# Second mixture-of-experts stage: one check of the routing search at the end instead of one per phase, and the low parts of w1 and w2 made by other engines and by adding DMAs

## The reference

```python
N, D, E, F = 3072, 512, 8, 1024
cap = N // E                                  # 384
logits = x @ w_gate                           # [N, E]
for idx in argsort(-logits.flatten()):        # all (token, expert) pairs, highest first
    tok, e = idx // E, idx % E
    if assigned[tok] >= 0 or counts[e] >= cap: continue
    assigned[tok] = e; counts[e] += 1
for e in range(E):
    mask = assigned == e                      # exactly 384 tokens
    out[mask] = np.maximum(x[mask] @ w1[e], 0) @ w2[e]
```

## Time and profile before

| | |
|---|---|
| time, median of 3 runs | 1040.14 us (1037.85 to 1042.40) |
| the profiled execution: time / span of the trace | 1041.54 us / 1039.8 us |
| attention and first mixture, up to 613 us | 613.0 us |
| start of routing 2, up to the first product | 44.4 us |
| windows 0 to 4 | 56.9, 52.1, 51.6, 51.6, 51.2 us |
| windows 5 and 6 | 38.3, 39.0 us |
| window 7 with the end | 41.7 us |
| PE busy in a window of about 51.6 us | 40.0 us |

### The profile page before, as it was taken

How to read it: one execution, slowest core, us unless ns; L and a number is a source line. 1 busy time by engine, 2 the same in 40 slices (tenths; PEclk the granted TensorE clock), 3 DMA queues, 4 the chain that set the end, 5 groups by cost and what they waited for, 6 DMA issues and landing times. The chain is left out here.

```text
span 1039.8 us, 18491 instructions
## 1 busy us (share of the span) xinstructions
PE 801.5 (77%) x5547; PEld 718.7 (69%) x5547; DVE 591.1 (57%) x1395; ACT 457.9 (44%) x1039; POOL 304.1 (29%) x314
## 2 busy tenths in 40 slices
PE   0588888878873599999999701759595959599996
PEld 0477877768773599999999601648484849487895
DVE  4475674774726366666666226776666676663430
ACT  0587885886850355555555101313131414143341
POOL 1101000010100202222222112354545455457762
PEclk9999999999895599999999955879798989899998
DMA  3988789688535355555553005052333333334320
GB/s 62 211 183 216 207 192 278 150 184 228 129 123 166 112 179 191 188 194 185 178 188 110 16 5 181 20 185 109 115 107 117 110 114 112 112 113 137 129 99 31
DMA packets 106920, 147.22 MB, mean 142 GB/s; under 512 B 35942, under 2 KB 63846, under 8 KB 106864
## 3 DMA queue, kind: packets, MB, share of 16 engines
q1 hardware_dynamic: 93232, 114.96, 39.5%
q0 software_dynamic: 7360, 18.96, 5.6%
q10 hardware_dynamic: 6272, 12.58, 3.2%
HBM read 125.86 MB, written 23.76 MB: 144 GB/s over the span
## 5 line engine op out<-in xcount | busy, mean ns | idle before, releaser
L1394 POOL TENSOR_TENSOR r_w2l<-r_w,r_w2h 128x512 fp32r<-128x512 f32 x64 | 99.1, 1560 | 50.1 <-ACT r_w2h L1573 49.9
L931 ACT ACTIVATE pr<-pr,nmx 128x232 f32<-128x232 f32 (+1 forms) x192 | 88.7, 464 | 13.0 <-DVE nmx L1006 11.7
L1487 PE MATMUL r_ph<-r_xh,r_w1h 128*128 128x384 f32 x256 | 88.4, 345 | 2.8 <-issue 2.7
L832 PE MATMUL sc<-kk,qh 128*128 128x256 f32 x192 | 60.6, 337 | 36.4 <-DVE ql L993 36.4
L844 PE MATMUL tp<-ident,pr 128*128 128x128 f32 x352 | 60.2, 292 | 35.7 <-ACT pr L931 35.6
L1487 PE MATMUL r_ph<-r_xl,r_w1h 128*128 128x384 f32 x256 | 86.5, 338 | 0.0
L1487 PE MATMUL r_ph<-r_xh,r_w1l 128*128 128x384 f32 x256 | 86.5, 338 | 0.0
L360 PE MATMUL m_ph<-m_xh,m_w1h 128*128 128x256 f32 x288 | 84.1, 292 | 0.9 <-issue 0.9
L1499 PE MATMUL r_py<-r_w2h,r_hh 128*128 128x512 f32 x192 | 83.0, 432 | 2.2 <-POOL r_w2l L1394 2.2
L360 PE MATMUL m_ph<-m_xh,m_w1l 128*128 128x256 f32 x288 | 81.7, 284 | 0.0
L360 PE MATMUL m_ph<-m_xl,m_w1h 128*128 128x256 f32 x288 | 81.7, 284 | 0.0
(11 more groups left out here) (245 smaller groups left out, 2239.9 us busy)
## 6 DMA issues: line engine op xcount, KB each, us to landing
m_w<-moe_w SPq DMA_DIRECT2D x18, 2048.0 KB, 9.3
r_w<-moe_w SPq DMA_DIRECT2D x32, 512.0 KB, 5.3
r_w<-moe_w SPq DMA_DIRECT2D x8, 2048.0 KB, 9.3
q_raw<-qT SPq DMA_DIRECT2D x32, 384.0 KB, 5.6
x_rows<-xb ACTq DMA_DIRECT2D x8, 1536.0 KB, 9.0
k_raw<-kT SPq DMA_DIRECT2D x64, 160.0 KB, 4.4
k_raw<-kT SPq DMA_DIRECT2D x64, 120.0 KB, 4.5
vo<-vL SPq DMA_DIRECT2D x16, 384.0 KB, 3.6
```

Of the source, the lines that this page charges most:

```text
L832: nc.tensor.matmul(to, qh[s][:, hh, q], kk[s][:, hh, keys], start=True, stop=False)
L931: nc.scalar.activation(pr[n % 4][:, t, lo:CW], pr[n % 4][:, t, lo:CW], ACT.Exp, bias=nmx[n % 4][:, t:t + 1], scale=-1.0, accum_out=sums[hd ...
L1394: g.tensor_tensor(w2l[:, m, :], w2[:, m, :], w2h[:, m, :].bitcast(F32), ALU.subtract).then_inc(w2_low, 1)
L1487: last = nc.tensor.matmul(ph[m % 4][:, 0:CAP], w[:, c, m * P:(m + 1) * P], x[:, c, :], start=(c == 0 and a == 0), stop=(c == KC - 1 and a ...
```

## The change

- `flag`, `bar` and `branch` with the exact search inside each phase go. `take_over` takes the bar directly; `close` gains two small operations (`least`, `astray`). After the last window every engine waits for `verdict` and loads `good`; only if it is 0 does the whole search and all eight experts run again, exactly (`general`, with windows 8 to 15). With `astray` set the scatters of the first pass go nowhere (`homes`, one more operation of 3 columns in `listing`).
- The attempts of phase f move from the y part of window f − 2 to the h part of window f − 1, in finer positions, called slots here: slot 2m + 1 is the end of block m of the h part, slot 16 + n is position n of the y part. Counts at 1, 5, 9, polls at 2, 6, 10, `total` at 12, `places` at 15, `table` at 23, `turn` at 34. In window 6: 5, 13 and 24 for the last three.
- w2l: ACT writes −w2h (`scale=-1.0`, rounded) into w2l behind each w2h, two chunks behind each of the first four blocks of h; POOL issues four DMAs of 512 KB that add w2 onto w2l in SBUF (`accum_op=add`).
- w1l: all four chunks on DVE, before the low parts of x. ACT makes all four high parts of w1 before it keeps y.
- SP loads w2 of window k only when the tokens of window k are gathered.

```diff
+            COUNT, POLL = (1, 5, 9), (2, 6, 10)
+            TOTAL, PLACES, TABLE, TURN = 12, H_SLOTS - 1, H_SLOTS + 7, H_SLOTS + 18
+            LAST_PLACES, LAST_TABLE, LAST_TURN = 5, 13, H_SLOTS + 8
...
+            def again(eng, passed_here, general):
+
+                eng.wait_ge(verdict, 1)
+                settle(eng, passed_here)
+                is_good = eng.value_load(good[0:1, 0:1])
+                with eng.If(is_good < 1):
+                    general()
...
+                def load1(k, e):
+                    if k:
+                        sp.wait_ge(w1_high, KC * k)
+                        sp.wait_ge(w1_low, KC * k)
+                    for c in range(KC):
+                        sp.dma_start(w1[:, c, :], w1b[bass.ds(e, 1), c * P:(c + 1) * P, :].rearrange("o p n -> p (o n)")).then_inc(w1_loaded[c], 16)
+
+                def load2(k, e):
+                    if k:
+                        sp.wait_ge(w2_high, FC * k)
+                        for i in range(FC // 2):
+                            sp.wait_ge(w2_low[i], 16 * k)
+                    sp.wait_ge(gathered, 16 * TT * (k + 1))
+                    sp.dma_start(w2[:], w2b[bass.ds(e, 1)].rearrange("o (c p) n -> p (o c) n", p=P)).then_inc(w2_loaded, 16)
...
                                          bounds_check=N - 1, oob_is_err=False).then_inc(scattered, 16)
 
-                def w1_low_part(k):
-                    for c in w1_sides(k)[1]:
-                        pool.wait_ge(w1_high, KC * k + c + 1)
-                        g.tensor_tensor(w1l[:, c, :], w1[:, c, :], w1h[:, c, :].bitcast(F32), ALU.subtract).then_inc(w1_low_pool, 1)
-
-                def w2_low_part(k, m):
-                    pool.wait_ge(w2_high, FC * k + m + 1)
-                    g.tensor_tensor(w2l[:, m, :], w2[:, m, :], w2h[:, m, :].bitcast(F32), ALU.subtract).then_inc(w2_low, 1)
+                def w2_low_part(k, i):
+                    pool.wait_ge(w2_turned, FC * k + 2 * i + 2)
+                    settle(pool, passed_pool)
+                    g.dma_start(w2l[:, 2 * i:2 * i + 2, :].bitcast(F32), w2[:, 2 * i:2 * i + 2, :], accum_op=ALU.add).then_inc(w2_low[i], 16)
 
                 gather(0)
-                w1_low_part(0)
-                for k in range(E):
+                for k in WINDOWS:
                     if k:
                         scatter(k - 1, TT - 1)
-                    for m in range(FC):
-                        w2_low_part(k, m)
-                        if m == (FC - 1 if k == 0 else FC // 2) and k < E - 1:
...
+                def search_step(k, slot):
+
+                    f = k + 1
+                    if f < PHASES:
+                        for r in range(TRIES):
+                            if slot == COUNT[r]:
+                                count(f, r)
+                            if slot == POLL[r]:
+                                poll(f, r)
+                        if slot == TOTAL:
+                            total(f)
+                        if slot == PLACES:
+                            places(f)
+                        if slot == TABLE:
+                            table(f)
+                        if slot == TURN:
+                            turn(f)
+                    elif f == PHASES:
+                        if slot == LAST_PLACES:
+                            places(f)
+                        if slot == LAST_TABLE:
+                            table(f)
+                        if slot == LAST_TURN:
+                            turn(f)
 
                 pe.wait_ge(ended, 1)
...
+                def w2_part(k, m):
+                    if m == 0:
+                        act.wait_ge(w2_loaded, 16 * (k + 1))
                     nc.scalar.activation(w2h[:, m, :], w2[:, m, :], ACT.Copy).then_inc(w2_high, 1)
+                    nc.scalar.activation(w2l[:, m, :], w2[:, m, :], ACT.Copy, scale=-1.0).then_inc(w2_turned, 1)
...
+                def middle(k):
                     if k:
                         act.wait_ge(y_done, TT * k)
                     for m in range(FC):
-                        if m == 0:
-                            act.wait_ge(w2_loaded, 16 * (k + 1))
                         h_high_part(k, m)
-                        w2_high_part(k, m)
+                        if m < FC // 2:
+                            w2_part(k, 2 * m)
+                            w2_part(k, 2 * m + 1)
+
+                def before_products(k):
+                    if k:
+                        act.wait_ge(h_done, FC * k)
+                    for c in range(KC):
+                        w1_part(k, c)
+
+                before_products(0)
+                for c in range(KC):
-                        act.wait_ge(h_done, FC * (k + 1))
-                        for c in (0, 1):
-                            w1_high_part(k + 1, c)
+                        before_products(k + 1)
                     y_keep(k, 0)
+                    y_keep(k, 1)
                     if k < E - 1:
                         for c in range(KC):
                             x_high_part(k + 1, c)
-                        for c in (2, 3):
-                            w1_high_part(k + 1, c)
-                    for t in range(1, TT):
-                        y_keep(k, t)
+                    y_keep(k, 2)
...
+                def take(f):
+
+                    v.tensor_tensor(taken[:], hot[:], cmpb[:].unsqueeze(2).broadcast_to(shape), ALU.mult).then_inc(chosen, 1)
+                    link(v.scalar_tensor_tensor(out=pen[:], in0=cmpb[:], scalar=-SPAN_OUT, in1=pen[:], op0=ALU.mult, op1=ALU.min))
+                    own()
+
+                def take_over(f):
+
+                    link(v.tensor_tensor(cmpb[:], bestm[:], cur[-1][:].broadcast_to([P, NT]), ALU.is_ge))
+                    take(f)
 
                 def close(f):
 
@@ -1727,16 +1713,25 @@
                     link(v.tensor_reduce(cnt[:], sums.rearrange("p (t e) -> p e t", e=E), AX.X, ALU.add))
                     link(v.tensor_tensor(left[:], left[:], cnt[:], ALU.subtract))
                     link(v.tensor_scalar(shut[:], left[:], 0.5, None, ALU.is_lt))
+                    link(v.tensor_reduce(least[:], left[:], AX.X, ALU.min))
+                    link(v.tensor_scalar(astray[:], least[:], -0.5, float(N), ALU.is_lt, ALU.mult))
...
+                        attempt(f, 1)
+                        h_low_part(k, 1)
+                        h_low_part(k, 2)
+                        judge(f, 1)
+                        settle_on(f, 1)
+                        attempt(f, 2)
+                        h_low_part(k, 3)
+                        h_low_part(k, 4)
                         judge(f, 2)
-                        h_low_part(k, 1)
                         settle_on(f, 2)
-                        flag(f)
-                        bar(f)
-                        h_low_part(k, 2)
-                        h_low_part(k, 3)
+                        take_over(f)
+                        h_low_part(k, 5)
                         close(f)
-                        h_low_part(k, 4)
-                        h_low_part(k, 5)
+                        pick_expert(f)
+                        h_low_part(k, 6)
+                        h_low_part(k, 7)
                         slots(f)
-                        h_low_part(k, 6)
                         marks(f)
-                        h_low_part(k, 7)
                         listing(f)
-                    elif f < PHASES:
-                        bar(f)
+                        bests()
+                        if f + 1 < PHASES:
+                            needs()
+                            attempt(f + 1, 0)
+                        else:
+                            check_all()
+                    elif f == PHASES:
...
-                        settle_on(k + 2, 0)
-                        attempt(k + 2, 1)
-                        judge(k + 2, 1)
-                        settle_on(k + 2, 1)
-                        attempt(k + 2, 2)
-                    if k < E - 1:
+                    if f < E:
                         for c in range(KC):
-                            x_low_part(k + 1, c)
-                    if k + 2 < PHASES:
-                        judge(k + 2, 2)
-                        settle_on(k + 2, 2)
-                        flag(k + 2)
-                    if k < E - 1:
-                        w1_low_part(k + 1)
+                            w1_low_part(f, c)
+                        for c in range(KC):
+                            x_low_part(f, c)
```

More of the change, by code:

```diff
@@ L51 @@
 TRIES = 3
-SPAN_OUT = 3e38
+SPAN_OUT = 1.6e38
 OPEN_BIG = 1e6
@@ L1409, in _, with general @@
                 scatter(E - 1, TT - 1)
+                def general():
+                    for k in AGAIN:
+                        gather(k)
+                        for i in range(FC // 2):
+                            w2_low_part(k, i)
+                        for t in range(TT):
+                            scatter(k, t)
+                    pool.wait_ge(scattered, 16 * TT * 2 * E)
```

(26 more changed lines are left out.)

398 lines of the change are left out of this document (185 added, 213 removed).

## The result

The kernel after takes 984.7 us (median of 4 runs, 983.8 to 987.7), the kernel before 1040.7 (4 runs, 1037.9 to 1042.4); the ratio is 0.947, 95% interval 0.944 to 0.950. The forecast was 984.0. The profiled execution is the slowest of the four, 987.7 us with a span of 986.0. Its stretches (from:to, length, then busy time and instructions of PE, PEld, DVE, ACT, POOL, the granted clock, DMA share, GB/s), to be read beside the earlier trace rows: the start of routing 2, windows 0, 2, 6 and 7, and the end.

A forecast was written before the change was run, and what follows sets the result against it. POOL's vector work holding DVE was taken to bound the kernel, afterwards a w2 loop of 25.6 + 9.3 + 6.3 = 41.2 us per window. Span 978.4, 978.7 in time, plus 5 for clock drops gave 984 us, range 975 to 994.

The forecast's parts named there:

- The bound before and the lever: Kernel before: POOL's subtractions hold DVE's `r_bestm` 8.66 us, PE idles 11.25 us before a count; 14 us per window lost.
- The loop: Windows 1 to 5: gather landed 25.6 us past poll 1, w2 load 9.3, landing to poll 1 6.3; period 41.2 us.
- The search's matmuls: In the h part: 0.68 us per count, poll 1's slot at 8.75 us, PE's own bound 37.4 us per window.
- The clock term: Behind PE waits of 2 us or more in six windows, half clock costs 1.5 us, about every second twice; 5 us.
- rival 4: Gather issues on POOL held up by DVE's w1l work, loop 2.4 us longer in six windows: 998 us; chance 0.05.
- The trap of the Trainium skill: At the gather issues: POOL cannot write its DMA descriptors while a two-port DVE operation runs; cited for the 2.4 us.
- The adding DMAs: POOL's DMAs making w2l cost PE nothing: no wait up to 4.0 us per transfer, 3.3 in window 7.
- R: Time per 512 KB adding DMA in SBUF, taken as 3.0 us, for two source reads; bounds 1.5 to 14.4 us.
- 5.1 + 4R: Time from w2's landing until a window's last adding DMA is there, four transfers summed; PE wants it at y position 6.
- The sum: Start, window 0, five windows of 41.2 us, windows 6 and 7 (37.9, 33.05), end 8.6: span 978.4 us without clock drops.

The follow-up runs named there:

- e1: The kernel before with only the low parts changed: w2l by negated ACT copies and adding DMAs, all w1l on DVE; 997.9 us, ratio 0.959 to before.
- e2: The changed kernel with w2l again made by eight POOL subtractions, no negated ACT copies; 989.0 us, ratio 0.949 to before.
- e5: The changed kernel with ACT's copies of w2 behind blocks 1 to 4 of h instead of 0 to 3; 972.5 us, ratio 0.932 to before.
- e9: The changed kernel with two spare ACT copies per window, behind blocks 0 and 1 of h; 999.5 us, ratio 0.965 to before.
- e4: The changed kernel with ACT's copies of w2 behind blocks 2 to 5 of h instead of 0 to 3; 986.3 us, ratio 0.947 to before.
- e8: The changed kernel without the test behind the last window and its code for a second search; 999.8 us, ratio 0.959 to before.
- e6: The changed kernel without SP's wait for the gather ahead of the w2 load; 986.2 us, ratio 0.945 to before.

## Why the prediction was right

**The bound before and the lever: shown.** e1 alone, which only takes the vector work off POOL, brings 44 of the 58 us of the stage. What exactly holds DVE for so long is not: e2, with w2l back on POOL, loses only 8.8 us.

**The loop: shown, part by part.** Forecast and trace: load 9.3, 9.6 us; landing to PE past poll 1 6.3, 6.0; from there to the third gather issue 21.9, 21.7; landed 3.6, 3.9; period 41.2, 41.4 in three windows of five and 42.1 in two (a load of 10.45 us in one, a gather held by DVE in the other). DVE's last low part of x ends 28.8 us behind poll 1 (forecast 28.9), ACT's first copy of y starts 20.8 behind it (20.5). e5 and e9 move the copies' stretch and the window follows.

**The search's matmuls were mis-sized.** I took 0.68 us for a count's 24 matmuls. With what it costs the products around it, it is 0.9, and the polls, which I had at next to nothing, add to it: poll 1's slot stands at 9.4, not 8.75, so PE waits there for 1.3 us in most windows and not 2.1, and its bound per window is 39.1, not 37.4. That mattered little for the period, which the loop sets, but for the next term.

**The clock term failed in size.** I took 5 us for drops in about half of the windows. The trace has none in windows 1 to 5, even behind the one wait of 2.2 us, and 1.6 us lost in window 6, where turn waited 1.95 us. PE's timeline has the turn,

```profile
928.26 2.03 PE L1473 MATMUL r_ph<-ident,r_xg 128*128 128x128 f32 x12 [1.95 <-DMA r_xg<-x_rows,rows]
```

and the chain the rest of the y part:

```profile
930.29 11.35 PE r_py L1498 x45
```

12 transposes in 2.03 us instead of 1.53 and 45 matmuls in 11.35 instead of 10.25. The mechanism and its price (1.5 us a drop) were right, as e9 shows, where every window, with waits of 2.08 to 3.6 us, had it.

**Window 6 had one more miss.** Its two last gather issues, beside `r_w1l` on DVE, took 1.96 and 1.93 us; in windows 0 to 4 `needs` and `attempt` stand on DVE in front of `r_w1l`, so that only the third issue meets it (1.55 us). POOL's timeline, window 6 and then window 2:

```profile
921.61 1.96 POOL L1399 DMA_INDIRECT r_xg<-x_rows,rows  x1 [0.30 <-issue]
923.87 1.93 POOL L1399 DMA_INDIRECT r_xg<-x_rows,rows  x1 [0.31 <-issue]
...
765.74 1.04 POOL L1399 DMA_INDIRECT r_xg<-x_rows,rows  x1 [0.30 <-issue]
767.08 1.55 POOL L1399 DMA_INDIRECT r_xg<-x_rows,rows  x1 [0.30 <-ACT r_yo L1607]
```

That is rival 4, in windows 5 and 6 instead of in six: PE's turn came 0.9 and 1.3 us later by it. The trap of the Trainium skill named in the prediction (SBUF — State Buffer, § SBUF: two separate sides) is about two-port operations of DVE and has POOL locked out while one runs; here the issues beside `r_w1l` were 0.5 to 0.9 us longer. So the trace agrees in direction, and whether this subtraction is such an operation no run shows.

**The adding DMAs: right.** R is 2.8 us for 3.0. But what decides is the latency: 5.1 us in the median, up to 6.3, and up to 7.4 in e4 for the last one of a window, which has a w1 load beside it, at issues 2.4 us apart. My term "5.1 + 4R" summed transfers that in fact overlap with the copies; it gave no wait, and none came, but e5 and e4 show that the margin was about one block of h (e5 waits once, 0.3 us) and less than two.

**The sum.** Span forecast without the clock 978.4, measured 986.0: routing 2 started 2.0 us later, window 0 was 1.9 shorter, windows 1 to 5 were 2.4 longer, window 6 2.2, the end 2.7, rest 0.2. So the median's 984.7 beside 984.0 owes something to luck: a clock term of 5 us, of which 1.6 came, stands for an end of 2.7 us and gather issues that I had at nothing, and a window 0 that was shorter by 1.9 us, thanks to a load of 8.1 us instead of 9.3, offsets a start that was later by 2.0.

## What to carry to other kernels

Follow the resource that is reloaded once per iteration around its whole loop (asked for, landed, converted, decided, asked for again) and add up its latencies; where the sum exceeds PE's own time, this is the period, and only a piece of that chain is worth moving, as far as to the next consumer's deadline and no further (e4, e5). And a PE wait near 2 us should be priced with the clock behind it: where it fell, 1.5 us more in most cases here and 2.7 in one.

## What was not expected of the hardware

- A DVE operation held up by POOL's vector work waited for one POOL operation (up to 1.2 us) in e2 and at some places of the kernel before, but for five in a row at others, 8.66 and 9.22 us.
- The granted clock fell from the level of 2.4 to that of 1.2 GHz behind PE waits of 1.65 and 1.67 (e2), 1.95 (after), 2.12 (e8), 2.13 (e4), 2.26 (e6) and 2.27 us (e8) and most longer ones, but not behind 1.95 (e4), 2.20 (after) and 2.72 us (e8). What decides between them no run shows.
- The 2 MB loads of the first mixture, whose code is the same in all kernels, took 9.1 to 9.3 us in the five programs without the test at the end and 8.1 to 8.4 in the eight with it.
- 512 KB from SBUF to SBUF: 1.3 us of the 16 engines and 2.9 us to landing as a plain copy, 2.8 and 5.1 us as an adding one; POOL issues it in 0.85 to 1.0 us.
- The end of the program is 2.7 us longer in every kernel in which POOL issues such DMAs.
